# Attention and feed-forward on one core: the reciprocals of the row sums spread by transfers through a DRAM scratch, TensorE's attention written out, new orders

## The reference

```python
q_rot, k_rot = rotate(q), rotate(k)
scores = (1 / sqrt(64)) * q_rot @ k_rot.T
scores = scores - max(scores)
attn = exp(scores); attn = attn / (sum(attn) + 1e-09)
x = (attn @ v) laid out as tokens x 512
h = x @ w_in
out = (max(h, 0) + alpha * min(h, 0)) @ w_out
```

## Time and profile before

| what | us |
|---|---|
| median of 3 runs | 677.0 (671.92, 677.0, 677.43) |
| the profiled execution's own time | 672.58 |
| its span, first to last instruction | 670.8 |
| TensorE busy in the span | 656.0 (98%) |
| VectorE (DVE) | 338.8 (51%) |
| ScalarE (ACT) | 320.7 (48%) |
| GpSimd (POOL) | 266.8 (40%) |

### The profile page before, as it was taken

The page is one execution under the profiler, slowest core; times in us unless marked ns, Lnnn a source line. Parts: engine busy times, 40 slices in busy tenths (PEclk is TensorE's granted clock), DMA queues, the critical chain, the costliest instruction groups (busy, mean ns, idle before and its releaser), DMA issues.

```text
span 670.8 us, 15166 instructions
## 1 busy us (share of the span) xinstructions
PE 656.0 (98%) x5570; PEld 561.7 (84%) x5570; DVE 338.8 (51%) x779; ACT 320.7 (48%) x730; POOL 266.8 (40%) x254
## 2 busy tenths in 40 slices
PE   8899999999999998999999999999999999999998
PEld 7677787777877776898899999999999999999996
DVE  4687777767888764445522332233233323332222
ACT  2788888868888875333332223222322232223223
POOL 3766788858865323222222222222222222222222
PEclk9999999989999999999999999999999999999999
DMA  6596554444554336000010001000100010001001
GB/s 148 153 229 178 124 136 110 106 105 103 120 121 104 83 117 251 1 1 1 1 48 0 1 1 47 1 1 0 47 0 0 0 47 0 0 0 48 1 0 48
DMA packets 73311, 41.62 MB, mean 62 GB/s; under 512 B 59812, under 2 KB 64292, under 8 KB 72740
## 3 DMA queue, kind: packets, MB, share of 16 engines
q1 hardware_dynamic: 72978, 40.62, 23.1%
q10 hardware_dynamic: 274, 0.16, 0.1%
HBM read 22.95 MB, written 4.72 MB: 41 GB/s over the span
## 4 chain that ended last, share of the span: by engine, by line
PE 94%; ACT 2%; DVE 1%; issue 1%; DMA 0%; SPq 0%; POOL 0%; ACTq 0%; DVEq 0%
PE banks L753 30%; PE banks L782 30%; PE banks L697 9%; PE banks L595 8%; PE banks L671 5%; PE banks L622 3%; PE banks L693 3%; PE banks L644 2%; PE banks L569 2%; PE banks L649 1%; ACT prob L824 1%; ACT pt L867 1%; DMA cos_sb<-in_cos 0%; PE banks L577 0%; PE banks L652 0%
## 5 line engine op out<-in xcount | busy, mean ns | idle before, releaser
L517 POOL TENSOR_TENSOR g_lo<-g,g_hi 128x384 fp32r<-128x384 f32 (+1 forms) x98 | 99.7, 1018 | 309.2 <-ACT g_hi L936 299.8
L1100 DVE TENSOR_SCALAR g<-banks,alpha_sb 128x384 f32<-128x384 f32 (+1 forms) x98 | 59.7, 610 | 250.9 <-ACT pos L927 250.9
L753 PE MATMUL banks<-x_hi,w_in_lo 128*128 128x384 f32 x384 | 129.3, 337 | 0.0
L753 PE MATMUL banks<-x_hi,w_in_hi 128*128 128x384 f32 x384 | 129.2, 337 | 0.0
L753 PE MATMUL banks<-x_lo,w_in_hi 128*128 128x384 f32 x384 | 129.0, 336 | 0.0
L927 ACT ACTIVATE pos<-banks 128x384 f32<-128x384 f32 x96 | 47.1, 491 | 170.2 <-PE banks L753 170.2
L782 PE MATMUL banks<-w_out_hi,g_hi 128*128 128x512 f32 x288 | 114.9, 399 | 0.3
L782 PE MATMUL banks<-w_out_hi,g_lo 128*128 128x512 f32 x288 | 112.9, 392 | 0.0
L782 PE MATMUL banks<-w_out_lo,g_hi 128*128 128x512 f32 x288 | 111.9, 388 | 0.0
L936 ACT ACTIVATE g_hi<-g 128x384 fp32r<-128x384 f32 (+1 forms) x98 | 50.9, 519 | 115.9 <-DVE g L1103 115.9
L824 ACT ACTIVATE prob<-prob,nmax 128x576 f32<-128x576 f32 x128 | 98.2, 773 | 1.3 <-DVE prob L991 1.2
(11 more groups left out here) (80 smaller groups left out, 917.3 us busy)
## 6 DMA issues: line engine op xcount, KB each, us to landing
q_swap<-q_nat SPq DMA_DIRECT2D x32, 256.0 KB, 3.7
k_swap<-k_nat SPq DMA_DIRECT2D x32, 144.0 KB, 3.1
out<-stage SPq DMA_DIRECT2D x18, 256.0 KB, 2.0
raw_q<-in_q SPq DMA_DIRECT2D x32, 128.0 KB, 2.9
raw_k<-in_k SPq DMA_DIRECT2D x32, 128.0 KB, 2.5
raw_v<-in_v SPq DMA_DIRECT2D x32, 128.0 KB, 2.3
w_in_raw<-in_moe_w_in SPq DMA_DIRECT2D x4, 1024.0 KB, 5.8
w_out_raw<-in_moe_w_out SPq DMA_DIRECT2D x8, 512.0 KB, 7.5
```

Of the source, the lines that this page charges most:

```text
L517: nc.gpsimd.tensor_tensor(g_lo[f % 2][:, part], g[f % 2][:, part], g_hi[f % 2][:, part].bitcast(F32), ALU.subtract).then_inc(g_lo_done, 1)
L753: mm = nc.tensor.matmul(h_ps[f % 2], w[:, j, cols], xx[:, j, :], start=(step == 0), stop=(step == 3 * CT - 1))
L1100: nc.vector.tensor_scalar(g[f % 2][:, part], h_ps[f % 2][:, part], 0.0, alpha_sb[:, f:f + 1], ALU.min, ALU.mult).then_inc(neg_done, 1)
```

## The change

The inverse sums go to a DRAM scratch `inv_dram` of 9 x 128 numbers in one transfer (`spread_inverse`, element by element) and come back in four, each a row of it broadcast to the 64 partitions of a head (`take_inverse`). Both are issued by SP: the first at the start of its period, ahead of `load(p + 2, 0)`, the other four between `load_v` and `load(p + 2, 1)`, after a wait for the first. Unit INV is gone, and MIXED has only q's and k's left rows. The reciprocals stand at the end of DVE's period. TensorE's attention is written out in place of its loop; the other engines keep theirs. The orders in `period` on TensorE, ACT and DVE are new, and four copies change their engine: KQREM, PB1, PB3 and PA2 go to ACT, PB2 and PA1 to DVE. The normalisation of the last pair moves into the first chunk of the feed-forward.

```diff
-U_INV = 10
-U_PA = (11, 12, 13, 14)
-UNITS = 15
+U_PA = (10, 11, 12, 13)
+UNITS = 14
 T_BANKS = 4
-BANK_OF = (1, 2, 3, 0, 1, 2, 3, 0, 1, 2, 2, 0, 1, 2, 0)
+BANK_OF = (1, 2, 3, 0, 1, 2, 3, 0, 1, 2, 0, 1, 2, 0)
...
+        inv_dram = nc.dram_tensor("inv_dram", (TILES, P), F32, kind="Internal").ap()
...
+            def spread_inverse(p, par):
+                if has_prev(p):
+                    sp.wait_ge(inv_done, p)
+                    sp.dma_start(inv_dram.rearrange("n c -> c n"), inv[:, par, :],
+                                 allow_slow_non_contiguous=True).then_inc(inv_out, 16)
+
+            def take_inverse(p):
+                if has_prev(p):
+                    sp.wait_ge(inv_out, p * 16)
+                    if not (isinstance(p, int) and p == 1):
+                        sp.wait_ge(x_done, (p - 1) * 2)
+                    for h, r in enumerate(HEADS):
+                        own = inv_dram[1 + h * QT:1 + (h + 1) * QT, :].rearrange("n c -> (n c)")
+                        sp.dma_start(inv_sb[r, 0:QT * P], own.unsqueeze(0).to_broadcast([D, QT * P])).then_inc(inv_in, 16)
+                        sp.dma_start(inv_sb[r, QT * P:S],
+                                     inv_dram[0, r].unsqueeze(0).to_broadcast([D, REM])).then_inc(inv_in, 16)
...
                     p = b * PAIRS + t
+                    spread_inverse(p, (t - 1) % 2)
                     if has_pair(p + 2):
                         load(p + 2, 0)
                     if not is_opening(p):
                         load_v(b, t)
+                    take_inverse(p)
                     if has_pair(p + 2):
                         load(p + 2, 1)
...
+                if f == 4:
+                    spread_inverse(PERIODS, (PERIODS - 1) % 2)
+                elif f == 8:
+                    take_inverse(PERIODS)
...
             def period(b, t):
 
                 p = b * PAIRS + t
+                score(p, t, REM_TILE)
                 spread(p, t, U_KQREM)
-                score(p, t, REM_TILE)
                 turn(p, t, U_QREM)
                 turn(p, t, U_KREM)
+                score(p, t, A_TILES[0])
                 turn_two(p, t, U_PB[0])
-                score(p, t, A_TILES[0])
                 score(p, t, A_TILES[1])
+                score(p, t, A_TILES[2])
                 turn_two(p, t, U_PB[2])
                 if not is_opening(p):
                     turn(p, t, U_Q)
                 if not is_opening(p):
                     turn(p, t, U_K)
-                score(p, t, A_TILES[2])
                 score(p, t, A_TILES[3])
-                if not is_opening(p):
-                    spread(p, t, U_MIXED)
+                score(p, t, B_TILES[0])
                 pv(b, t, 0)
                 if not has_now(p):
                     hidden(0, 0, 0)
-                score(p, t, B_TILES[0])
                 score(p, t, B_TILES[1])
...
-                spread(p, t, U_INV)
+                score(p, t, B_TILES[2])
+                if not is_opening(p):
+                    spread(p, t, U_MIXED)
                 turn_two(p, t, U_PA[0])
-                score(p, t, B_TILES[2])
                 score(p, t, B_TILES[3])
-                turn_two(p, t, U_PA[2])
                 pv(b, t, 1)
                 if not has_now(p):
                     hidden(0, 0, 1)
+                turn_two(p, t, U_PA[2])
...
-            batches(pe, batch)
+            for b in range(NB):
+                batch(b)
             period(NB, 0)
```

ACT's steps in an ordinary period, after: copies KQREM, QREM, KREM, PB0, PB1, exp REM, copy PB3, exp A0, high Q, high K, exp A1, A2, A3, high MIXED, exp B0, copy PA0, exp B1, B2, B3, copies PA2, PA3. DVE's: maxima REM, A0, A1, A2, copy PB2, maxima A3, B0, low Q, low K, maxima B1, normalise 0, low MIXED, maxima B2, B3, normalise 1, copy PA1, and the reciprocals of this pair:

```diff
-                    dve.wait_ge(evac[BANK_OF[U_INV]], evac_count(p, U_INV))
+                    dve.wait_ge(inv_in, p * 4 * 16)
...
-                normalise(p, *before, 1)
+                if has_now(p):
+                    normalise(p, *before, 1)
+                flat(p, U_PA[1], t)
+                if has_now(p):
+                    reciprocals(p + 1, t + 1, 0)
+                if has_now(p):
+                    reciprocals(p + 1, t + 1, 1)
...
+                        if f == X_AT[0] - 2:
+                            for h in range(2):
+                                normalise(PERIODS, NB - 1, PAIRS - 1, h)
```

More of the change, by code:

```diff
@@ L272, in build @@
         inv_done = sem("inv_done")
+        inv_out, inv_in = sem("inv_out"), sem("inv_in")
         pv_done = sem("pv_done")
@@ L631, in spread @@
                     pe.wait_ge(exp_done, (p - 1) * TILES + 1)
-                elif u != U_INV and has_next(p):
+                else:
                     turned_in(p, 1)
-                if u != U_KQREM and has_prev(p):
-                    pe.wait_ge(inv_done, p)
                 pe.sem_inc(pair_filled, 1)
-                par = (t - 1) % 2
                 if u == U_KQREM:
@@ L640, in spread @@
                         mm = nc.tensor.matmul(bank[r, 0:REM], prob_rem[:, QT * P:S], ident[:, r], start=True, stop=True)
[L641 to L645, removed]
-                else:
[L647 to L652, removed]
-                                                  ident[:, r], start=True, stop=True)
+                else:
+                    for r in HEADS:
+                        mm = nc.tensor.matmul(bank[r, 0:P], rot_q[:, QT, r], ident[:, :], start=True, stop=True)
                 mm.then_inc(turned, 1)
@@ L861, in flat @@
                     jobs = [(pt_half(t % 2, u), half_bank(bank))]
-                else:
-                    if not (isinstance(p, int) and p == 1):
-                        act.wait_ge(x_done, (p - 1) * 2)
-                    jobs = [(inv_sb[:, 0:QT * P], bank)]
                 for dst, src in jobs:
@@ L880, in period @@
                 flat(p, U_PB[0], t)
+                flat(p, U_PB[1], t)
                 exps(p, t, REM_TILE)
-                flat(p, U_PB[2], t)
+                flat(p, U_PB[3], t)
+                exps(p, t, A_TILES[0])
                 if not has_now(p):
@@ L890, in period @@
                     hi(p, U_K, t)
-                exps(p, t, A_TILES[0])
-                if not is_opening(p):
-                    hi(p, U_MIXED, t)
                 exps(p, t, A_TILES[1])
@@ L899, in period @@
                         hi(p, u, t)
-                flat(p, U_INV, t)
+                if not is_opening(p):
+                    hi(p, U_MIXED, t)
                 if not has_now(p):
@@ L1019, in lo @@
                                                              op0=ALU.mult, op1=ALU.subtract)
-                if u == U_MIXED and has_prev(p):
-                    ins = nc.vector.tensor_copy(inv_sb[:, QT * P:S], bank[:, P:P + REM])
                 ins.then_inc(evac[BANK_OF[u]], 1)
@@ L1109, in period @@
                 before = (b if t else b - 1, (t - 1) % PAIRS)
-                reciprocals(p, t, 0)
-                flat(p, U_KQREM, t)
                 maxima(p, t, REM_TILE)
-                reciprocals(p, t, 1)
-                flat(p, U_PB[1], t)
                 maxima(p, t, A_TILES[0])
                 maxima(p, t, A_TILES[1])
-                flat(p, U_PB[3], t)
                 maxima(p, t, A_TILES[2])
+                flat(p, U_PB[2], t)
+                maxima(p, t, A_TILES[3])
+                maxima(p, t, B_TILES[0])
                 if not is_opening(p):
                     lo(p, U_Q, t)
-                if not is_opening(p):
-                    lo(p, U_K, t)
-                maxima(p, t, A_TILES[3])
-                if not is_opening(p):
-                    lo(p, U_MIXED, t)
                 if not has_now(p):
@@ L1128, in period @@
                         split_x(0, 0, j)
-                maxima(p, t, B_TILES[0])
+                if not is_opening(p):
+                    lo(p, U_K, t)
                 maxima(p, t, B_TILES[1])
@@ L1133, in period @@
                         lo(p, u, t)
-                normalise(p, *before, 0)
+                if has_now(p):
+                    normalise(p, *before, 0)
                 if not has_now(p):
@@ L1138, in period @@
                     gate(0, 0, 0)
+                if not is_opening(p):
+                    lo(p, U_MIXED, t)
                 maxima(p, t, B_TILES[2])
                 maxima(p, t, B_TILES[3])
-                flat(p, U_PA[2], t)
-                normalise(p, *before, 1)
+                if has_now(p):
[3 more added lines that the diff above has]
+                    reciprocals(p + 1, t + 1, 0)
+                if has_now(p):
+                    reciprocals(p + 1, t + 1, 1)
             nc.vector.memset(blank[:, :], 0.0).then_inc(blank_done, 1)
```

22 lines of the change are left out of this document (8 added, 14 removed).

## The result

| | us |
|---|---|
| median of 4 runs after | 800.39 (798.73 to 804.68) |
| before, on the same chip | 676.97 |
| ratio after / before | 1.1875 (1.1829 to 1.1922); 1.182 by the two medians alone |
| the profiled execution's own time, its span | 799.51, 797.7 |

Predicted were 676 us, with a range of 661 to 692. The change costs 123 us, far outside. The page after shows where: the span, the granted clock in 40 slices, the largest queue, and the chain that ended last by engine and by line.

A forecast was written before the change was run, and what follows sets the result against it. TensorE, at 94% of the span, bounds the kernel; the inverse's loop through SP would then set 15.1 us a period. Terms +2.4 + 2.6 - 1.3 - 4.0 - 0.5 = -0.8 us, giving 676 us, range 661 to 692.

The forecast's parts named there:

- the landing of the spread: Transfer of inverse sums to DRAM: 72 elements per DMA engine at 27.7 ns plus a store's 2.0 us, landing at 4.0 us.
- The estimate that the prediction took from the Trainium skill: Spread to DRAM: if read-modify-write below 512 B doubled each element's time, landing at 6.0 us, adding 0.2 us a period.
- Rival C: Spread lands after 5.8 us, SP waits at inv_out with broadcasts, load k and swaps behind; 691 us, chance 0.28.
- R to X: From the reciprocals' end (R) to the last broadcast's landing (X), through SP's queue: 10.1 us, bounds 9.0 and 12.
- X to R: From the last broadcast's landing through normalise 0, pv 1, normalise 1, copy, addition and reciprocal to the next R: 5.0 us.
- SP's issues: SP's queue from the reciprocals' end to the last broadcast's issue: spread, load q, load_v, broadcasts, 7.5 us.
- POOL's slack: K's rotation on POOL, slack 4 us, near zero left after MIXED's move; costs nothing, at worst 0.35 us in eight periods.
- TensorE's code written out: TensorE's attention loop: writing it out removes the loop's turn, -4.0 us, bounds 0 and -4.0.
- the price of the new order on TensorE: Score tiles in five blocks and pv twice between other work: about two more changes of kind, 0.3 us a period.
- TensorE's bound of 14.05 us: Period TensorE alone would need without L644 and L652 and with the new order's extra crossings, against 14.86 before.
- the loop and its order of links: Closed chain from reciprocals through SP's transfers, normalise and pv 1 to the next reciprocals: 15.1 us a period, against 14.86 before.
- ACT's and DVE's moved copies: Copies exchanged between engines have cover on both: ACT 12.8 of 14.05 us a period, DVE 10.6.

The follow-up runs named there:

- e6: Changed kernel with SP's order altered: load q first, then the 4-byte spread, its wait and the broadcasts before load_v; 805.59 us.
- e10: e6's order, inverse by rows of 9, plus a second, unread spread of 512 dense 4-byte pieces that is waited for; 800.84 us, one run.
- e9: e6's order, inverse by rows of 9, plus a second, unread spread of 1,152 4-byte pieces 64 B apart that is waited for; 708.75 us, one run.
- e8: Kernel before with the 4-byte spread added at the head of SP's period, its result used by nobody; 777.48 us.
- e1: Changed kernel with the spread written as 128 rows of 9 numbers (36 bytes) in place of 1,152 4-byte pieces; 704.14 us.
- e5: Changed kernel with rows of 9 and SP's order load q, spread, its wait and broadcasts, then load_v; 691.12 us.
- e13: e5 without two of the four v transfers of batches 1 to 3 (head 1's values stay old); 681.79 us.
- e7: Changed kernel without the scratch, the inverse back on TensorE (INV ahead of B1, last 64 columns in MIXED), new orders and written-out code kept; 677.72 us.
- e3: Kernel before with only TensorE's batches written out in place of the loop; 669.35 us.
- e14: e9 with the second spread's 1,152 pieces 16 B apart in place of 64 B; 719.95 us, one run.
- e16: e8's control: kernel before with the same unused spread, written in rows of 9 in place of 4-byte pieces; 678.67 us.

## Why the prediction was wrong

**The step that failed is the landing of the spread**: "72 x 27.7 = 2.0 us, with the 2.0 us of a store 4.0 us", bounds 2.0 and 7.0. It took 10.7 us with nothing behind it (e6), 12.4 and 10.1 in the two periods shown of after. I priced a write of 4 bytes by the packets of loads, "the nearest rows", and took the count as what it scales with. The nearest rows were of another kind: reads of 256 bytes from DRAM into partitions of their own. e10 and e9 show that the count is hardly the scale, so no price per element, at 27.7 or 70 ns, could have given it. The same 1,152 pieces at a pitch of 64 bytes wait 3.3 us and land in 3.7 (e9), close to the predicted 4.0: the number was right for pieces that don't share a stretch of memory, and nothing in the trace of before spoke of those that do.

The estimate that the prediction took from the Trainium skill ("DMA: Bandwidth & Descriptors", Rules for kernel authors and Specifications), 6.0 us by one descriptor per element and a read-modify-write below 512 B, fares as follows. One descriptor per element: the runs agree, with their 1,024 packets per spread more than rows of 9. The doubling for pieces under 512 B was the prediction's own guess: such pieces took 3.7 us at 64 bytes' pitch and 10.7 dense, and rows of 36 bytes 2.1, so the length of a piece alone does not tell which it is.

**Rival C was the mechanism, its price too small.** It had SP wait at the broadcast for the spread, with broadcasts, load k and swaps behind it, and 691 us at a landing of 6.5. Its sum comes out with the measured landing: 12.4 us is 6.6 past the 5.8 that were covered, 10.1 + 6.6 = 16.7, and R to X was 16.9. With X to R at 7.7 that makes the loop 24.6; over eight middle periods (102.51 to 292.86) it is 23.8, some 9 us more than 14.86, in 14 periods 125 us. Measured: 123. That the sum fits so well is in part luck. C had SP standing at the wait, with the issues ahead of it at their usual length. In after SP stood there for 18.5 us in all, because those issues were drawn out until the spread had nearly landed. In e6, with nothing between the spread and the wait, SP stood 141.6 us, and the time was the same. And in e8 nobody waits for the inverse, and 103 us are lost all the same, on the loads, on pauses and on the clock. So the same sum can be reached by either way; the two overlap and don't add.

**SP's issues were sized too small**, "0.1 + 0.65 + 0.1 + 2.5 + ... = 7.5 us": with the spread quick (e1) they took 8.6 on average in the eight middle periods, and X - R was 11.5, late but inside the bound of 12; the period shown, with 9.8 and 12.5, is past it. I costed SP only between R and X and did not ask for its whole period: five more transfers bring it to 13.6 us of issuing (e5), and with the wait of 3.0 us for the spread on top that is more than TensorE's 14.05. e13 fits this bound.

**X to R, 5.0 us, became 6.4 on average in e1, and 7.6 in the period shown**, in two terms. pv 1 was taken at 2.55, its time before; it took 3.6 on average, 4.3 in this period. And the addition of 0.43 us took 0.75 on average, here 1.27. This window of e1 covers this pv 1 (columns as above):

```profile
129.70:133.90 4.20, 4.20 (x22) 2.00 (x22) 1.92 (x7) 1.63 (x4) 4.12 (x5) 0.61 0.73 187
```

0.61 granted, where the 11.6 us before it, the wait of 2.67 us among them, had 1.00. Of the eight middle periods five had pv 1 at 3.8 to 5.1 us and a clock of 0.50 to 0.68, each behind a stand of 2.0 to 3.2 us; three had 2.64 us and 1.00, two of them behind stands of 0.9 and 1.5 us, but one behind 2.85. So the low clock came only behind the longer stands, and not behind all of them. The prediction wrote "TensorE stands for a us in front of pv 1" and had no term for a slower pv 1.

**POOL's slack**, "Cost nothing, at worst 0.35 us in each of the eight periods with weight splits": in e7 these periods are some 0.5 us longer than the others of the new order, 4 of the 8.4 us. I had found the slack near zero and then took the better end of the range. The other 4 to 5 us are TensorE's 0.3 us a period, which the sum had.

Two slips in the working change nothing: 14.86 - 1.13 + 0.3 is 14.03, not 14.05, and in rival C a landing of 6.5 us makes X - R 10.8, not 10.95.

**Right were**: TensorE's code written out, -4.0 predicted and -5.0 measured (e3); the price of the new order on TensorE, 0.3 us and 0.33 (e7); TensorE's bound of 14.05 us without the inverse, 14.1 and 14.0 in e1's last periods; the loop and its order of links; that ACT's and DVE's moved copies cost little (in e7 TensorE waits for a copy five times in the whole kernel, 3.8 us in all). Put together by measured steps: 674.3 before (677.0 beside after), -5 for the written-out code (669.4), +8.4 for the orders (677.7), +26 for the way through DRAM in place of TensorE (704.1), +96 for the layout of the scratch (800.4). The forecast's sum of -0.8 had -4 for the first; by its 0.3 us a period some +5 for the second, which leaves some -2 for the third; and nothing for the fourth.

## What to carry to other kernels

Don't write the words of many partitions one by one, side by side, into DRAM: write each partition's numbers as one row, or turn them first. Look also at what is queued behind a slow transfer: here it was late as well, even where nobody read the slow one. Before a queue of issues gets more work, add up its whole period, not only the stretch on the path. A unit of TensorE that costs 1.1 us of 14.9 is cheap against a path of 10 us through two landings. The gain in this change was in its plainest line, the loop written out, and that alone is the kernel to keep (669.35 us).

## What the runs showed of the hardware

- A write of 512 or 1,152 single words, dense in DRAM, lands after 9.8 (e10) or 10.7 us (e6). 1,152 words at 16 bytes' pitch take 4.4 us (e14), at 64 bytes' pitch 3.7 (e9), and the same numbers as rows of 36 bytes 2.1 (e1).
- While it is under way the issue of a following transfer can take up to 4.9 us (after) or 7.1 us (e8) in place of 0.4 to 0.6, and a small load issued behind it landed 12.3 us later (e8), though in after's 11.6 us behind a spread (124.4 to 136.0) the DMA engines are on average 56% busy at 30 GB/s:

```profile
124.40:136.00 11.60, 8.21 (x114) 5.85 (x112) 3.60 (x9) 6.85 (x16) 3.56 (x3) 1.00 0.56 30
```

- TensorE, too, has pauses in these kernels for nothing that the profile names, 37.7 us in e8 against 4.3 in e16, as here in e8 at 128.04 (in brackets the idle time before it). The page lists a DMA queue of the kind "instruction" (42 packets, 0.69 MB); that TensorE waits for its own instructions there is argued, not shown.

```profile
128.04 0.27 PE L657 MATMUL banks<-ident,inv 128*64 128x128 f32 x1 [0.89 <-issue]
```

- DVE's addition of 9 columns takes from 0.16 to 1.31 us in e1 and after. In all 18 cases of 0.3 us or more a POOL instruction ends 0.02 to 0.03 us before it does. In e1:

```profile
135.06 1.27 DVE L1052 TENSOR_TENSOR rsum<-rsum,tiny 128x9 f32<-128x9 f32 x1
```

```profile
134.84 1.47 POOL L489 TENSOR_TENSOR w_in_hi<-w_in_raw,zero 128x768 f32 x1
```

136.33 against 136.31 us; after, 148.61 against 148.59. Which of the two holds the other up no run here separates.
